# One product for turning and routing attention's outputs, and a new order at two stage borders, in an attention, expert and mixing kernel

## The reference

```
q_bits, k_bits = (q @ proj > 0), (k @ proj > 0)          # 6 bits; equal buckets may attend
scores = where(q_bucket == k_bucket, q @ k.T / 8, -1e9)
attn   = exp(scores - max); attn /= sum + 1e-9
x      = attn @ v, heads side by side                      # (2, 768, 512)

logits = x @ w_gate; local = sigmoid(x @ w_local)          # 8 experts
e      = argmax(logits) where local < 0.5, else the expert of the token before
x      = softmax(logits)[e] * (relu(x @ w1[e]) @ w2[e])

theta  = x @ w_theta; zr, zi = x * cos(theta), x * sin(theta)
u      = x + w_tok_r @ zr + w_tok_i @ zi                   # over tokens
out    = u + relu(u @ w_ch)
```

## Time and profile before

| | |
|---|---|
| median of 3 runs | 695.04 us (694.35 to 700.62) |
| the profiled execution | 690.3 us, of which the span from the first to the last instruction is 688.5 us |
| PE busy | 625.6 us (91%) |
| DVE, ACT, POOL busy | 399.9, 350.0, 244.5 us |
| mean granted clock of TensorE | 0.968 |

### The profile page before, as it was taken

How to read it: one execution, slowest core, us unless ns; L and a number is a source line. 1 busy time by engine, 2 the same in 40 slices (tenths; PEclk the granted TensorE clock), 3 DMA queues, 4 the chain that set the end, 5 groups by cost and what they waited for, 6 DMA issues and landing times. The chain is left out here.

```text
span 688.5 us, 10408 instructions
## 1 busy us (share of the span) xinstructions
PE 625.6 (91%) x3701; PEld 495.3 (72%) x3702; DVE 399.9 (58%) x731; ACT 350.0 (51%) x524; POOL 244.5 (36%) x198
## 2 busy tenths in 40 slices
PE   3899999999999996398999999999278999999998
PEld 1666677676667673298799899989166888878886
DVE  6767777777777663763444355332278867732422
ACT  3767767767767771553454355331355765420200
POOL 5752707254361000355633663360335532200000
PEclk9999999999999998589999999999789999999999
DMA  9204260707254503799847755510552002421201
GB/s 295 88 1 123 115 208 31 260 9 253 66 195 157 181 11 106 265 368 352 293 162 250 254 204 195 213 60 21 181 186 78 16 1 92 151 94 48 90 31 61
DMA packets 57263, 99.23 MB, mean 144 GB/s; under 512 B 16896, under 2 KB 23040, under 8 KB 57216
## 3 DMA queue, kind: packets, MB, share of 16 engines
q1 hardware_dynamic: 54848, 91.00, 38.6%
q0 software_dynamic: 2080, 6.82, 2.7%
q10 hardware_dynamic: 288, 0.79, 0.3%
HBM read 69.23 MB, written 29.36 MB: 143 GB/s over the span
## 5 line engine op out<-in xcount | busy, mean ns | idle before, releaser
L388 DVE TENSOR_REDUCE scores<-scores 128x1 f32<-128x768 f32 x96 | 92.7, 966 | 41.7 <-PE scores L503 40.5
L329 ACT COPY probs_t<-turned 128x768 f32<-128x768 f32 x96 | 76.7, 799 | 62.4 <-PE turned L512 62.1
L919 POOL TENSOR_TENSOR w_lo<-stage,w_hi 128x1024 fp32r<-128x1024 f32 x28 | 76.3, 2756 | 78.5 <-ACT w_hi L914 73.6
L337 ACT ACTIVATE probs<-scores,bias,scale 128x768 f32<-128x768 f32 x96 | 95.4, 994 | 12.8 <-DVE bias L395 12.5
L512 PE MATMUL turned<-ident,probs 128*128 128x128 f32 x576 | 79.7, 275 | 5.1 <-ACT probs_t L329 5.1
L512 PEld LDWEIGHTS turned<-ident,probs 128*128 128x128 f32 x576 | 67.4, 141 | 14.4 <-issue 11.6
L1027 PE MATMUL up<-xt_hi,w_hi 128*128 128x256 f32 x256 | 73.7, 288 | 3.5 <-DVE xt_lo L971 2.0
L1027 PE MATMUL up<-xt_lo,w_hi 128*128 128x256 f32 x256 | 73.4, 287 | 0.0
L524 PE MATMUL pv<-probs_t,v_in 128*64 128x384 f32 x384 | 72.3, 498 | 0.9 <-ACT probs_t L329 0.9
L1027 PE MATMUL up<-xt_hi,w_lo 128*128 128x256 f32 x256 | 73.1, 286 | 0.0
L503 PE MATMUL scores<-k_aug,q_aug 76*128 76x384 f32 x192 | 60.1, 395 | 7.6 <-DVE k_aug L381 5.1
(11 more groups left out here) (170 smaller groups left out, 1240.9 us busy)
## 6 DMA issues: line engine op xcount, KB each, us to landing
stage<-in_w SPq DMA_DIRECT2D x64, 512.0 KB, 4.6
x_slots<-zeros SPq DMA_DIRECT2D x7, 1024.0 KB, 8.3
y_slots<-zeros SPq DMA_DIRECT2D x7, 1024.0 KB, 10.2
wt_raw<-in_w_tok SPq DMA_DIRECT2D x9, 768.0 KB, 4.3
q_raw<-in_qT SPq DMA_DIRECT2D x16, 384.0 KB, 5.2
k_raw<-in_kT SPq DMA_DIRECT2D x14, 384.0 KB, 6.1
x_in<-x_slots SPq DMA_DIRECT2D x9, 512.0 KB, 5.4
y_slots<-y_out SPq DMA_DIRECT2D x8, 512.0 KB, 4.6
```

The source lines that it names most:

```text
L329: nc.scalar.copy(probs_t[j % 2][:, a, :, t % 3 * P:(t % 3 + 1) * P].rearrange("k (b n) q -> k b n q", b=2), turned[:, :, 0:HALF].rearrange ...
L337: nc.scalar.activation(probs[g % 3][:].rearrange("p (b n) -> p b n", b=2), scores[g % 2][:, :, 0:HALF], ACT.Exp, bias=bias[:, pair, a, t:t ...
L388: nc.vector.tensor_reduce(neg_max[g % 2], scores[g % 2][:, :, 0:HALF], AX.XY, ALU.max, negate=True).then_inc(s_neg, 1)
L919: name.tensor_tensor(w_lo[w][:, r, :], stage[:, r, :], w_hi[w][:, r, :].bitcast(F32), ALU.subtract).then_inc(done, 1)
```

## The change

In attention, the routing weights `w_heads` become the last 18 columns of a tile `w_turn`, whose first 128 columns are the identity matrix, copied there by one more operation of POOL. For j = 0 to 14, `turn_out(j)` makes one float32 product of 146 columns for each tile instead of a product of 18 and a transpose. For j = 15 the product of 18 columns is made for the three tiles first, into the PSUM tile of the scores, with a semaphore of its own (`s_hl`) for `normalise_logits`, and the three transposes follow. `turn_out(14)` moves ahead of the products of the loop's step g = 98; before, it followed at g = 100.

In experts, each half of `y_out` is stored by its own transfer of 256 KB as soon as DVE has copied it.

In mixing, ACT and DVE split `w_theta` in two halves, and ACT does so before it loads its table for the sine. SP issues the first load of token weights only once the first gathered tile has landed. On DVE `x_low(0)` stands before `gated(1)`; `gated(3)` to `gated(11)` go to ACT, behind `turn(c)`; `columns_low(1)` moves from c = 0 to c = 1, behind `x_low(2)`.

```diff
-    done(nc.gpsimd.memset(route.w_heads[:], 0.0))
+    done(nc.gpsimd.memset(route.w_turn[:, :, P:TURNED], 0.0))
+    done(nc.gpsimd.tensor_copy(route.w_turn[:, :, 0:P], ident[:].unsqueeze(1).to_broadcast([P, NPAIRS // B, P])))
...
-            for n in range(3):
-                nc.tensor.matmul(head_logits[:, n * 2 * (E + 1):(n + 1) * 2 * (E + 1)], out_t[j % 2][:, n * P:(n + 1) * P],
-                                 route.w_heads[:, j // 2 % 4, :, :].rearrange("p a e -> p (a e)"), start=True, stop=True)
-            for n in range(3):
-                last = nc.tensor.transpose(side[:, n * P:(n + 1) * P], out_t[j % 2][:, n * P:(n + 1) * P], ident[:])
+            if j < PARTS_OF_PAIRS - 1:
+                for n in range(3):
+                    last = nc.tensor.matmul(turned_out[:, n, :], out_t[j % 2][:, n * P:(n + 1) * P],
+                                            route.w_turn[:, j // 2 % 4, :], start=True, stop=True)
+            else:
+                for n in range(3):
+                    last = nc.tensor.matmul(last_logits[:, n * 2 * (E + 1):(n + 1) * 2 * (E + 1)],
+                                            out_t[j % 2][:, n * P:(n + 1) * P], route.w_turn[:, j // 2 % 4, P:TURNED],
+                                            start=True, stop=True)
+                last.then_inc(s_hl, 1)
+                for n in range(3):
+                    last = nc.tensor.transpose(turned_out[:, n, 0:P], out_t[j % 2][:, n * P:(n + 1) * P], ident[:])
             last.then_inc(s_ot, 1)
...
+            if g == STEPS + 2:
+
+                side_free(LAST_BUT_ONE)
+                turn_out(PARTS_OF_PAIRS - 2)
             for m in (g - PV_LAG, g - PV_LAG + 1):
                 if 0 <= m < STEPS:
                     products(*divmod(m, 6))
...
-            sp.wait_ge(s_y, 2 * g + 2)
-            sp.dma_start(y_rows[bass.ds(g, 1), :, :, :].rearrange("a p j d -> (a p) j d"), y_out[:]).then_inc(s_out, 16)
+            for j in range(2):
+                sp.wait_ge(s_y, 2 * g + j + 1)
+                sp.dma_start(y_rows[bass.ds(g, 1), :, j, :].rearrange("a p d -> (a p) d"), y_out[:, j, :]).then_inc(s_out, 16)
...
-            if i == 1:
-                sp.wait_ge(s_whi, 1)
-                sp.wait_ge(s_wlo, 1)
+            if i == 0:
+
+                sp.wait_ge(s_g[0], 16)
+            elif i == 1:
+                sp.wait_ge(s_whi, 2)
+                sp.wait_ge(s_wlo, 2)
...
+        def gated(c):
+            act.wait_ge(s_g[c], 16)
+            act.wait_ge(s_gated, c)
+            nc.scalar.activation(x_tok[:, c, :], x_tok[:, c, :], ACT.Copy, scale=gate[:, c:c + 1]).then_inc(s_gated, 1)
...
+        act.wait_ge(s_wraw, 16)
+        for half in range(2):
+            high(wm_hi[:, 2 * half:2 * half + 2, :], w_raw[:, 2 * half:2 * half + 2, :], s_whi)
         act.wait_ge(s_c, 2)
         nc.scalar.activation(sine[:], half_pi[:], ACT.Sin).then_inc(s_sine, 1)
-        act.wait_ge(s_wraw, 16)
-        high(wm_hi[:], w_raw[:], s_whi)
...
             turn(c)
+            if c + 3 < NC:
+                gated(c + 3)
             if c >= 1:
                 waves(c - 1)
...
-        dve.wait_ge(s_whi, 1)
-        low(wm_lo[:], w_raw[:], wm_hi[:], s_wlo)
+        for half in range(2):
+            at = slice(2 * half, 2 * half + 2)
+            dve.wait_ge(s_whi, half + 1)
+            low(wm_lo[:, at, :], w_raw[:, at, :], wm_hi[:, at, :], s_wlo)
         gated(0)
+        x_low(0)
         gated(1)
-        x_low(0)
         columns_low(0)
         gated(2)
...
-            if c + 3 < NC:
-                gated(c + 3)
+            if c == 1:
+                columns_low(1)
             if c >= 2:
                 z_low(c - 2)
             reduce_angle(c)
-            if c in (0, 2):
-                columns_low(1 + c // 2)
+            if c == 2:
+                columns_low(2)
```

More of the change, by code:

```diff
@@ L27 @@
 N_CONSTS = 20
-ROUTE_CONSTANTS = 24
+ROUTE_CONSTANTS = 25
 STICKY = -1.5 * 2.0 ** -23
@@ L31 @@
 NC = B * T
+TURNED = P + 2 * (E + 1)
 UNIT = 2 * P
@@ L56, in __init__ @@
         self.w_route = sb("w_route", [P, NPAIRS // B, E + 1])
-        self.w_heads = sb("w_heads", [P, NPAIRS // B, 2, E + 1])
+        self.w_turn = sb("w_turn", [P, NPAIRS // B, TURNED])
+        self.w_heads = self.w_turn[:, :, P:TURNED].rearrange("p k (a e) -> p k a e", a=2)
         self.parts = sb("parts", [P, NC, E + 1, H])
@@ L90, in routing_constants @@
     done(nc.gpsimd.iota(route.token_i[:, 1, :], pattern=[[0, NC]], base=0, channel_multiplier=1))
-    pool.wait_ge(s_route, 7)
+    pool.wait_ge(s_route, 8)
     done(nc.gpsimd.tensor_copy(route.slots[:], route.slot_i[:]))
@@ L150, in attention @@
     side = ctx.enter_context(nc.psum_tensor("side", [P, 512], F32))
-    head_logits = side[:, HALF:HALF + 3 * 2 * (E + 1)]
+    turned_out = side[:, 0:3 * TURNED].rearrange("q (t c) -> q t c", c=TURNED)
+    head_logits = [turned_out[:, :, P:TURNED].rearrange("q t (a e) -> q t a e", a=2) for j in range(PARTS_OF_PAIRS - 1)]
+    last_logits = scores[0][:, 0, 0:3 * 2 * (E + 1)]
+    head_logits.append(last_logits.rearrange("q (t a e) -> q t a e", t=3, a=2))
     s_const_ld = sem("s_const_ld")
@@ L177, in attention @@
     s_norm = sem("s_norm")
+    s_hl = sem("s_hl")
     s_route = sem("s_route")
@@ L416, in normalise @@
             tiles = slice(3 * half, 3 * half + 3)
-            nc.vector.tensor_tensor(x_of(pair, tiles), side[:, 0:HALF].rearrange("q (t a d) -> q t a d", t=3, a=2),
+            nc.vector.tensor_tensor(x_of(pair, tiles), turned_out[:, :, 0:P].rearrange("q t (a d) -> q t a d", a=2),
                                     recip[:, :, tiles].rearrange("q a t -> q t a").unsqueeze(3).to_broadcast([P, 3, 2, D]),
@@ L422, in normalise_logits @@
             pair, half = divmod(j, 2)
-            dve.wait_ge(s_ot, j + 1)
+            if j < PARTS_OF_PAIRS - 1:
+                dve.wait_ge(s_ot, j + 1)
+            else:
+                dve.wait_ge(s_hl, 1)
             dve.wait_ge(s_rec, 2 * pair + 2)
@@ L554, in on_the_side @@
                 project(pair + 1, range(2), n // K_AT, side)
-            if g >= TURN_LAG and (g - TURN_LAG) % 6 == 0 and (g - TURN_LAG) // 6 < PARTS_OF_PAIRS:
-                side_free(g)
-                turn_out((g - TURN_LAG) // 6)
+            if g >= TURN_LAG and (g - TURN_LAG) % 6 == 0 and (g - TURN_LAG) // 6 in range(PARTS_OF_PAIRS):
+                if g != LAST_BUT_ONE:
+                    side_free(g)
+                    turn_out((g - TURN_LAG) // 6)
+        LAST_BUT_ONE = 6 * (PARTS_OF_PAIRS - 2) + TURN_LAG
         for g in range(0, STEPS + TURN_LAG, 2):
@@ L888, in prologue @@
         def prologue():
-            sp.sem_inc(s_out, 16)
+            sp.sem_inc(s_out, 32)
             for r in range(NP):
@@ L990, in unit @@
             x_low(g + 1)
-            dve.wait_ge(s_out, 16 * g + 16)
+            dve.wait_ge(s_out, 32 * g + 32)
             dve.wait_ge(s_sc, 16 * NC)
@@ L1335, in _ @@
         z_low(NC - 1)
-        dve.wait_ge(s_whi, 2)
+        dve.wait_ge(s_whi, 3)
         low(wm_lo[:], w_raw[:], wm_hi[:], s_wlo)
@@ L1376, in angles @@
             if c == 0:
-                pe.wait_ge(s_wlo, 1)
+                pe.wait_ge(s_wlo, 2)
             if c >= 2:
@@ L1407, in channels @@
             if n == 0:
-                pe.wait_ge(s_wlo, 2)
+                pe.wait_ge(s_wlo, 3)
                 pe.wait_ge(s_r, 4 * NC)
```

6 lines of the change are left out of this document (4 added, 2 removed).

## The result

| | median of the runs | lowest to highest | profiled execution | its span |
|---|---|---|---|---|
| before | 695.71 us | 694.24 to 700.62 | 690.3 us | 688.5 us |
| after | 691.70 us | 686.0 to 697.44 | 689.82 us | 688.0 us |

The ratio after to before is 0.9914, with a 95% interval of 0.9889 to 0.9939: 6.0 us faster (4.2 to 7.7). It is taken over all fast executions, without one slow one of the kernel after (697.44 us), while the two medians alone are 4.0 us apart. Forecast were 8.0 us less and 687.0, in a range of 681.5 to 691.5. The ratio, taken from the forecast's own 695.04, gives 689.1, inside the range; the bare median of 691.70 lies 0.2 us outside of it. The gain is 0.9%: of the three outcomes the prediction gave 0.55 to "faster by over 1%", and the one that came, "within 1%", had 0.42.

The account below looks back on a forecast made before the run. PE was taken to bound attention and the time from 524 us, a chain over several engines the start of mixing. Terms -2.7 - 1.3 - 0.1 - 1.5 - 2.4 = -8.0 us gave 687.0 us, range 681.5 to 691.5.

Parts of the forecast that it names:

- turn_out, 13 times: Attention, j = 0 to 13: six passes of 146 columns take 0.74 us instead of 0.95; -2.7 us (0 to -2.9).
- POOL's extra copy: Attention: POOL's copy of 512 columns, 0.55 us, is covered by its waits and costs nothing.
- end of attention: Moving turn_out(14) ahead of the last products gives -1.3 us; for j = 15, logits before the transposes give -0.1.
- routing and experts, "moves as one": After attention: routing, a rigid chain of DVE, PE and POOL, shifts as one with the expert weights' loads.
- last store: End of experts: a last store of 256 KB lands sooner than 512 KB; PE's wait 1.5 us shorter (-1.2 to -1.5).
- start of mixing, gated(0): Start of mixing: earlier splitting of w_theta and a held load bring the first angles 1.5 us earlier (0.4 to 1.6).
- half clock in the first angles: Start of mixing: first angles, starting earlier, may see less of the full clock; 0.3 us more allowed.
- gated off DVE: Mixing, before the dense stretch of PE: two gated operations leave DVE's line, 1.2 us.
- Rival C: turn_out: identity product costs four times a transpose per column; slower than before, +1.9 us, 696.9 us; chance 0.04.
- Rival B: Attention: nothing gained inside, a pass takes 0.16 us or another engine bounds; -5.3 us, 689.7 us; chance 0.16.
- Rival A: Start of mixing gives its gain back through late held loads or a late sine; -5.6 us, 689.4 us; chance 0.17.
- Rival D: Clock: PE's half-clock time after a border shifts 2 us either way, worth 1 us each at experts and mixing; no chance given.

Follow-up runs that it names:

- e11: The whole change with 166 tiny PE instructions added at PE's start, as e6, run again on another chip: 684.67 us, ratio to before 0.9887.
- e9: The kernel before with 76 tiny PE instructions added at PE's start, placing experts' code where e6 has it: 691.70 us, ratio to before 0.9963.
- e7: The whole change, but the first load of token weights does not wait for the first gathered tile: 692.23 us, ratio to before 0.9956.
- e2: The kernel before with only the store of y_out in two halves: 694.12 us, ratio to before 0.9973.
- e6: The whole change with 166 tiny PE instructions added at PE's start: 686.11 us, ratio to before 0.9868.
- e5: The whole change with 90 tiny PE instructions added at PE's start, as many as the change took out: 688.24 us, ratio to before 0.9890.
- e10: The kernel before with 166 tiny PE instructions added at PE's start: 698.67 us, ratio to before 1.0071.
- e3: The kernel before with only the edits of mixing, the held load among them: 692.90 us, ratio to before 0.9936.
- e1: The kernel before with only the edits of attention, with w_turn and POOL's copy: 694.40 us, ratio to before 0.9978.
- e12: e11 with gated(3) to gated(11) kept on DVE: 685.72 us, ratio to before 0.9899.
- e8: The whole change, but gated(3) to gated(11) stay on DVE: 692.46 us, ratio to before 0.9967.
- e4: The whole change once more, beside its three parts on the same chip: 692.51 us, ratio to before 0.9925.

## Why the prediction was right, and which step of it failed

By the ratio the time fell in the range, and the sign was right. But what came is the sum of a gain somewhat smaller than forecast (6.3 us by the traces) and of a loss that the prediction didn't have; that these two together stayed within the range is in part luck. Step by step, what was forecast and what the traces show:

| step | forecast | found |
|---|---|---|
| turn_out, 13 times | -2.7 | attention as a whole -4.3 |
| POOL's extra copy | 0 | 0 |
| end of attention | -1.3 - 0.1 | (in the -4.3) |
| routing and experts, "moves as one" | 0 | +5.3 in this pair of profiles, +0.1 in e11 against e9 |
| last store | -1.5 | -0.9 |
| start of mixing, gated(0) | -1.5 | -1.5 |
| half clock in the first angles | +0.3 | +0.66 |
| gated off DVE | -1.2 | -0.3, what is left of mixing's 1.1 |

**Attention** went as the price of the pass said: 0.84 ns a column, six passes of 146 in 0.75 us where 0.74 stood. Rival C, four times a transpose for each column, is refuted: that would have been 1.5 us. The rule that the prediction sets against the rows there, from the Trainium skill, TensorE: Matmul & The Clock Gate, section Terms, does not hold here: a tile's product of 146 columns takes 0.25 us and a transpose of 128 columns 0.11, a factor of two for each column. Rival B, nothing gained in attention, is refuted too: 4.3 us.

**The step that failed** is "routing is a rigid chain of DVE, PE and POOL and moves as one, with the expert weights' loads". Routing and the loads do. But experts doesn't only run at another time; its code also stands in another place. The prediction doesn't count PE's instructions ahead of it, though the diff gives their number (90 less). Waits for issue there grew from 1.5 to 5.9 us, 4.4 us given back, and where the clock falls behind the wait 1.6 us more. Of the rest of the 5.3, 1.7 us are one load of x_in, waited for 3.5 instead of 1.8 us; with and without the change this wait goes from 1.2 (e7) to 3.8 us (e2, e6), so it is the single execution's. Against it stands a clock that rose earlier in the first unit (in the block it is at half for 3.4 instead of 6.1 us), worth 1.4 us. That the place is the cause of the waits was shown in both directions: restored place brings them back to before's one of 1.6 us (e5), another place leaves next to none (e6, e11), and the kernel before catches them by a shift alone (e10) and loses its own by another (e9).

How much of the median this takes is less sure. By its waits the whole change is 4.4 us dearer in its own place than in the kernel before's. By the times, e5 in the place of before came to -7.6 us and the change in its own to -6.0 and -5.2: 1.6 to 2.4 us, with intervals of about 3 us on such a difference. The kernel before loses more by a shift into the place one block behind that of the whole change: e10 takes 4.9 us more than it (2.9 to 7.0). The waits are the same in both executions of the whole change (5.9) and near each other in before, e2 and e3 (1.5, 1.7, 1.4), so I take the sign as shown and the size as open between 1.6 and 4.9. The lower end fits the whole change better: 6.3 us of gain less 1.6 is 4.7, within what was measured (4.2 to 7.7), and less 4.9 is not.

The trace ties the waits to the instruction queue, whose 30 packets hold 0.49 MB, 16 KB each. In the ten traces that have them, there are 16 waits for issue of over 1 us in experts, 1.4 to 3.9 us long. Only in seven does a packet start during the wait. But in all 16 PE goes on 3.9 to 4.9 us after the start of the last packet ahead of the wait (4.5 in the kernel after's first, 4.4 in its second). e1's first wait is shorter than that of the kernel after, 2.2 us against 3.7, at the same place and with DMA engines as full, and it is its packet that starts earlier: 2.2 us ahead of the wait instead of 0.8. What the profile doesn't show is why the block comes no sooner, nor what passes between the packet's recorded end, 0.9 to 1.5 us after its start, and PE's next product. That PE waits for a block of its code is thus argued; that the waits hang on the place of the code is shown. The Trainium skill, Runtime: NRT & Kernel Launch, section Instruction fetch mechanics, says that an engine's instructions are refilled in blocks of 16 KiB, and that a taken branch to a target outside of what is loaded makes it fetch before it can go on. The trace agrees: the packets have this size, and all 16 waits stand where the code branches, at the border between units. The price is the trace's own, and full DMA engines don't fix it: the waits in which they are full (share 0.97 to 1.05) take 1.4 to 3.9 us, those at a share of 0.03 to 0.25 take 1.8 to 2.2.

**The store** is worth some 0.9 us rather than 1.5, as the 3.5 us to landing of the earlier trace rows was a slow instance of one: in e1, e9 and e10 the whole store landed after 2.8, in e3 after 3.2. The half landed after 2.0, as forecast. The border without the halves takes 4.4 to 5.05 us in five traces, 4.5 in the middle one, against 3.6 with them (and 4.13 in e2). A single transfer was priced from a single row, and the same row of other executions would have said so.

**Mixing** began as forecast: gated(0) 4.0 us after the block's start, first angles at 7.3 (7.2 forecast). Then two terms were mis-sized. The first angles lie wholly at the half clock now, 5.46 us instead of 4.80: +0.66 instead of the 0.3 allowed. And taking `gated` off DVE frees little. The chain of e11 shows why:

```profile
490.67 8.57 DMA w_raw<-in_w_tok
...
515.09 2.77 DVE wt_lo L1305
...
518.61 2.98 PE theta L1412 x12
```

wt_lo(2) takes 2.77 us there, and 2.78 after, where 2.16 stood before, while the same operation takes 1.67 elsewhere (the chain counts only what the operation adds to it; the timeline has 2.86, 2.25 and 1.75). The timelines show what differs, first before, then after:

```profile
519.52 2.53 POOL L1172 TENSOR_TENSOR z<-z,x_tok 128x512 f32<-128x512 f32 x2 [4.97 <-ACT z L1223]
...
521.41 2.25 DVE L1265 TENSOR_TENSOR wt_lo<-wt_raw,wt_hi 128x1536 fp32r<-128x1536 f32 x1
```

```profile
517.83 2.53 POOL L1200 TENSOR_TENSOR z<-z,x_tok 128x512 f32<-128x512 f32 x2 [3.77 <-ACT z L1256]
...
519.11 2.86 DVE L1301 TENSOR_TENSOR wt_lo<-wt_raw,wt_hi 128x1536 fp32r<-128x1536 f32 x1
```

When DVE starts, POOL's second product with x has 522.05 - 521.41 = 0.64 us left before and 520.36 - 519.11 = 1.25 after, and the low part takes 0.50 and 1.11 us more than its 1.75. In all fourteen traces a low part that starts with 0.63 us left of such a product takes 2.24 to 2.26, with 1.25 left 2.85 to 2.87; one that starts ahead of the product takes 1.75, and the product is then the longer one (1.5 to 2.7 us for 1.3). So 0.6 of the 1.2 us come back in the very next low part, because it now starts just behind POOL's product, and on ACT a `gated` holds the engine for 0.7 us, not the 0.5 of the estimate. e12 against e11, 0.9899 against 0.9887 and 1.05 us by the medians, is within the intervals, and the traces of e8 and e12 point opposite ways: whether the move to ACT is worth anything stays open. Rival A had part of this: the held load of wt 0, issued at 493.56, was waited for until 499.32, 9.8 us after the block's start and beyond the 9.6 that I had named as the limit; and in e11 wt 1 took 8.57 us to land, 13.1 us after the block's start where the forecast had 10.5, with turn(0) queued behind its cast on ACT. But the block gains all the same: dense stretch at 33.2 where 32.0 was forecast and 34.3 stood before (e11: 32.5).

Together: -4.3 - 0.9 - 1.5 + 0.7 - 0.3 = -6.3 us, inside what e11 against e9 measures at equal place (-5.3 to -7.0 us by the times, -7.6 by the spans), where 8.0 was forecast. The mis-sized terms are the store (0.6 us) and the start of mixing (-1.1 instead of -2.4).

Rival D, the clock, was the right reason to widen the range, and is worth more than the 1 us each that it named at experts and mixing. e4 is the kernel after once more, and its span is 3.7 us longer (691.7) with the same waits for issue. In experts its clock is at half for 10.3 us instead of 3.4, and the block takes 201.70 us instead of 198.65; from mixing's first transposes to the first channel product it is 121.14 instead of 119.29. Single times of the kernel after go from 686.0 to 697.4.

## What to carry to other kernels

Whoever adds or removes instructions ahead of code with branches moves that code. Here 90 PE instructions were worth up to 7 us, as much as the change, so compare two versions at equal instruction counts ahead of the branch, or try a few paddings of each, before you credit a difference of 1% to an idea. In a profile such a wait is an idle stretch marked "issue" on the first instruction behind a branch, which ends 4 to 5 us after the start of a packet of the instruction queue, with no engine at work that could be its cause. And a term that rests on a single transfer or a single border should carry the spread of such events in other executions.

## What the hardware showed that I had not expected

- Waits of 1.4 to 3.9 us ahead of PE's products behind a branch, with the DMA engines full (3.8 us at a share of 1.02, 389 GB/s, in e10; 2.2 us at 1.01 in e1) or nearly idle (1.8 us at 0.03 in e10); PE goes on 3.9 to 4.9 us after the start of the last packet of its code ahead of them. The same kernel with more instructions (e6: 10528 in all) is faster than with fewer (10362), by some 3 us by the ratios (0.9868 to 0.9914).
- After such a wait of 3.8 us, half clock for 3.3 us in e10, with PE busy throughout, and after one of 2.2 us in e1 and in e4. After PE stood still for 3.7 us in the kernel after, none.
- DVE's low part of 1536 columns takes 1.75 us alone or when it starts ahead of POOL's product with x, 2.25 when it starts with 0.63 us of that product left, and 2.86 with 1.25 left.
